# Attention turns the reciprocals of its totals instead of its output and stores x by features

## The chip, the cores and the metric

One core of a Trainium2 chip runs the whole program in one launch. The metric is the device time of that core in microseconds. The engines named below are TensorE (PE in the rows, with PEld for its weight loads), VectorE (DVE), ScalarE (ACT), GpSimd (POOL) and SyncE (SP), which issues most of the DMAs.

## The reference, cut to what matters

Three layers follow one another; each takes the result of the one before.

```python
# attention: q, k, v are (4 batches, 8 heads, 576, 64)
scores = scale * (q @ k.T) + bias            # bias from positions, one map per head
attn = np.exp(scores - scores.max(-1))
attn = attn / (attn.sum(-1) + 1e-09)
out = attn @ v
# dense layer: x is (4*576 = 2304 tokens, 8*64 = 512 features)
x = out.transpose(0, 2, 1, 3).reshape(2304, 512)
h = x @ w_in                                 # 512 -> 2048
x2 = (h - np.tanh(h)) @ w_out                # 2048 -> 512
# experts: each token goes through the one expert of 8 that its gate picks
y = gate * (np.maximum(x2 @ w1[e], 0) @ w2[e])
```

The division by the sum of the exponentials (the *total* of a query and a head) and the layout of x between the first two layers are what this case is about.

## The kernel before

**Attention** works on 16 pairs of heads (g from 0 to 15), and in each on five tiles of queries (t from 0 to 4; four of 128 rows and one of 64), 80 steps in all. In a step TensorE computes the scores of the next tile (`scores`, L412), turns the exponentials of this one (`turn_prob`, L420) and multiplies with v for the pair before (`values`, L427). VectorE adds the bias and finds the maximum of each row (`add_bias`, L644, once for each of the two heads), copies turned exponentials out of PSUM (L713) and splits the next pair's q and k into high and low parts (`low`, L626 and L629). ScalarE takes the exponentials and sums them into `total` (`exponentials`, L563), copies the rest of the turned exponentials (L599, L601) and makes the high parts. There is one PSUM buffer of scores for each head, so `scores` of a tile waits until both `add_bias` of the tile before have read it (`neg_done`, L403 to L405). Each engine carries out its instructions in the order in which they are written.

The output of a pair stands in PSUM with its 128 features on partitions and the 576 queries in columns. VectorE copies it to `o_sb` (`copy_main` at t = 3, L672; `copy_rest` at t = 4, L678). TensorE turns it back tile by tile (`turn_out`, L458), so that queries are on partitions, and VectorE multiplies each turned tile with the reciprocals of the totals while it writes `x_sb` (`scaled`, L664). The reciprocals come from `inverse` (L649 to L654): an addition and a reciprocal on 128 partitions by 10 values (five tiles by two heads), once for each pair, at t = 1 of the pair after it, ahead of `scaled` and of the next `add_bias`. Tile 0 of a pair is turned and scaled at t = 4 of the next pair, and tiles 1 to 4 in steps 0 to 3 of the one after. SyncE stores each pair to `x_dram`, one row for each token (L368, L369).

**The dense layer** takes six chunks of 384 tokens. In each it goes through 16 slots: `up` (L985, 12 matmuls with w_in), an activation shared by ScalarE and VectorE, and `down` (L1042, 9 matmuls with w_out). It needs x with features on partitions, in a high and a low part. So x is loaded by rows (`load_x`, L889), TensorE turns it (`turn_first_x`, L929, for chunk 0 at the end of attention; `turn_x`, L1029, for the others in slots 0, 3 and 6 of the chunk before), and ScalarE and VectorE split it out of PSUM (L934, L939; L1142, L1230). At the change of layers the last pair's `inverse` stands on VectorE ahead of the split of chunk 0, and `first_up` (L989) waits for that split.

**The experts** follow; the change does not touch their arithmetic.

Of the kernel before, what the change touches and what calls it, by code (L numbers as in the profile page):

```python
# [26 lines left out]
P = 128  # L27
# [56 lines left out]
class Dense:  # L84
# [8 lines left out]
    turn_first_x: object  # L93
    split_first_x_high: object
    split_first_x_low: object
# [24 lines left out]
    turned: object  # L120
# [32 lines left out]
def bias_and_attention(nc, stay, mem, w1, b1, w2, dist, psi, rpsi_rows, bias_dram, q, k, v, ident, x_dram):  # L153
# [8 lines left out]

    with ExitStack() as ctx:
# [23 lines left out]
        x_sb = [buf(f"x_sb{i}", [P, QT, 2 * D]) for i in range(2)]  # L187
# [19 lines left out]
        inv = [buf(f"inv{i}", [P, QT, 2]) for i in range(2)]  # L207
# [31 lines left out]
        x4 = x_dram[0:TOK, :].rearrange("(b s) (c e) -> b c s e", b=NB, e=2 * D)  # L239
# [47 lines left out]
        def over(engine):  # L287

            engine.wait_ge(x_done, QT * PAIRS_A)
            for i in range(2):  # L290
                engine.wait_ge(x_out[i], 32 * PAIRS_A // 2)
# [10 lines left out]
        def sync(sp, dense):  # L302
# [45 lines left out]
            for g in range(PAIRS_A + 1):  # L348
# [11 lines left out]
                if g == LASTP:  # L360
                    sp.wait_ge(x_out[LAST_OF_FIRST % 2], 32 * (LAST_OF_FIRST // 2 + 1))
                    dense.load_x(sp, 0)
                    dense.load_second_weights(sp)
                if real(g - 2):
                    p = g - 2
                    sp.wait_ge(x_done, QT * (p + 1))
                    dst = x4[p % NB, p // NB]
                    sp.dma_start(dst[0:MAIN, :].rearrange("(t p) d -> p t d", p=P), x_sb[p % 2][:, 0:QT - 1, :]).then_inc(x_out[p % 2], 16)  # L368
                    sp.dma_start(dst[MAIN:S, :], x_sb[p % 2][0:LAST, QT - 1, :]).then_inc(x_out[p % 2], 16)  # L369
# [4 lines left out]
            sp.wait_ge(x_out[(LAST_OF_FIRST + 1) % 2], 32 * ((LAST_OF_FIRST + 1) // 2 + 1))  # L374
# [3 lines left out]
            dst = x4[p % NB, p // NB]  # L378
            sp.dma_start(dst[0:MAIN, :].rearrange("(t p) d -> p t d", p=P), x_sb[p % 2][:, 0:QT - 1, :]).then_inc(x_out[p % 2], 16)
            sp.dma_start(dst[MAIN:S, :], x_sb[p % 2][0:LAST, QT - 1, :]).then_inc(x_out[p % 2], 16)  # L380
            for i in range(2):
                sp.wait_ge(x_out[i], 32 * PAIRS_A // 2)

        def tensor(pe, dense):
# [94 lines left out]
            for g, t in STEPS:  # L479
# [22 lines left out]
                if turn_of(g, t):  # L502
                    turn_out(*turn_of(g, t), misc, TURN_AT)
# [5 lines left out]
            dense.turn_first_x(pe)  # L509
            misc_free(PAIRS_A, 0)  # L510
            for tile in range(1, QT - 1):
                turn_out(LASTP - 1, tile, misc, tile * P)
            pe.wait_ge(pta_read, QT * PAIRS_A)
            turn_out(LASTP - 1, QT - 1, pt_a, 0)
# [5 lines left out]
            for tile in range(QT - 1):  # L520
                turn_out(LASTP, tile, misc, tile * P)
            turn_out(LASTP, QT - 1, pt_a, 0)

        def scalar(act, dense):
# [83 lines left out]
            for j in range(CH):  # L608
                dense.split_first_x_high(act, j)
            dense.split_second_high(act)  # L610

        def vector(dve, dense):
# [36 lines left out]
            def inverse(p):  # L649
# [4 lines left out]
                nc.vector.reciprocal(inv[p % 2][:, :, :], guarded[:, :, :]).then_inc(norm_step, 1)  # L654

            def scaled(p, tile, tiles, bank, at):
                m = rows(tile)
                if tile <= 1 and p >= 2:
                    dve.wait_ge(x_out[p % 2], 32 * (p // 2))
                dve.wait_ge(norm_step, 2 * p + 2)  # L660
                dve.wait_ge(turn_done, QT * p + tile + tiles)
                by = inv[p % 2][0:m, tile:tile + tiles, :]
                by = bass.AP(by.tensor, by.offset, [by.ap[0], [2, tiles], [1, 2], [0, D]])
                nc.vector.tensor_tensor(x_sb[p % 2][0:m, tile:tile + tiles, :].rearrange("p t (c d) -> p t c d", c=2),  # L664
                                        bank[0:m, at:at + tiles * P].rearrange("p (t c d) -> p t c d", c=2, d=D),
                                        by, ALU.mult).then_inc(x_done, tiles)

            def copy_main(p):
                if p:
                    dve.wait_ge(turn_done, QT * p - 1)  # L670
# [3 lines left out]
            def copy_rest(p, bank, at):  # L674
                if p:
                    dve.wait_ge(turn_done, QT * p)
# [55 lines left out]
            for j in range(CH):  # L732
                dense.split_first_x_low(dve, j)
# [13 lines left out]
CH = 3  # L747
# [25 lines left out]
def dense_and_routing(nc, stay, mem, attention, ctl, first_ctl, slot_i, rows_sb, w_in, w_out, w_gate, before, token_ids, down_order, upto,  # L773
# [4 lines left out]
    with ExitStack() as ctx:  # L778
# [50 lines left out]
        first_turn = [h.rearrange("p (k t) -> p k t", t=P) for h in halves[0:CH]]  # L829
# [7 lines left out]
        x_in = [sem(f"x_in{j}") for j in range(CH)]  # L837
        turned, xt_high, xt_ready = sem("turned"), sem("xt_high"), sem("xt_ready")
# [48 lines left out]
        x_tiles = x_dram[0:TOK, :].rearrange("(c t p) n -> c p t n", p=P, t=CH)  # L887
# [27 lines left out]
        def load_second_x(sp):  # L915
            sp.wait_ge(turned, CH)
# [8 lines left out]
        def turn_first_x(pe):  # L925
            for j in range(CH):
                pe.wait_ge(x_in[j], 16)
                for k in range(KT):
                    last = nc.tensor.transpose(first_turn[j][:, k, :], x_nat[:, j, k * P:(k + 1) * P], id_sb[:, :])  # L929
                last.then_inc(turned, 1)  # L930

        def split_first_x_high(act, j):
            act.wait_ge(turned, j + 1)
            nc.scalar.activation(xt_hi[0][:, :, j * P:(j + 1) * P], first_turn[j][:, :, :], ACT.Copy).then_inc(xt_high, 1)  # L934

        def split_first_x_low(dve, j):
            dve.wait_ge(xt_high, j + 1)
            cols = slice(j * P, (j + 1) * P)
            nc.vector.tensor_tensor(xt_lo[0][:, :, cols], first_turn[j][:, :, :], xt_hi[0][:, :, cols].bitcast(F32),  # L939
# [53 lines left out]
        def sync(sp, experts):  # L993
# [11 lines left out]
            for c in range(CHUNKS):  # L1005
                if c + 2 < CHUNKS:
                    sp.wait_ge(turned, CH * (c + 2))
# [12 lines left out]
        def tensor(pe, experts):  # L1020
            def turn_x(c, j):
                n = c * CH + j
                pe.wait_ge(x_in[j], 16 * (c + 1))
                if n:
                    pe.wait_ge(xt_ready, n)
                if j == 0 and c >= 3:
                    pe.wait_ge(x2_copied, CH * (c - 2))
                for k in range(KT):
                    last = nc.tensor.transpose(turn[:, k, :], x_nat[:, j, k * P:(k + 1) * P], id_sb[:, :])  # L1029
                last.then_inc(turned, 1)  # L1030

# [40 lines left out]
            for m in range(SLOTS):  # L1072
# [5 lines left out]
                j = x_prep(m)  # L1078
                if j is not None:
                    if m == 0:  # L1080
                        attention.turned(pe)
                    turn_x(m // FT + 1, j)
                j = x2_turn(m)
                if j is not None:
                    if j == 0:
                        if m // FT < LATE:
                            pe.wait_ge(xt_ready, CH * (m // FT + 2))
# [51 lines left out]
        def scalar(act, experts):  # L1139
            def split_x(c, j):  # L1140
                act.wait_ge(turned, c * CH + j + 1)
                nc.scalar.activation(xt_hi[c % 2][:, :, j * P:(j + 1) * P], turn[:, :, :], ACT.Copy).then_inc(xt_high, 1)  # L1142

# [877 lines left out]
```

## Time and profile before

| | us |
|---|---|
| median of three runs | 1080.85 |
| lowest and highest | 1079.69, 1084.35 |
| the profiled execution | 1080.45 |
| its span in the trace | 1078.7 |
| TensorE busy | 1037.8 (96%) |
| VectorE busy | 680.2 (63%) |
| ScalarE busy | 626.1 (58%) |

The setup of the bias takes the first 62 us or so, attention goes up to about 356, the dense layer up to about 795 (the first expert's work begins in its last slots), and the experts take the rest. Times in a timeline are microseconds from the start of the span. A value in square brackets behind a row is the time that the engine sat idle before it, and what ended that.

### The profile page before, as it was taken

The page shows a single profiled execution, that of the slowest core. Times are in us where ns is not written, and L with a number is a line of the kernel's source. Part 1 is how long each engine was busy: PE and PEld are TensorE (multiplying, and loading weights), DVE is VectorE, ACT ScalarE, POOL GpSimd, SP SyncE. Part 2 cuts the span into 40 slices and gives each one's busy share as a digit, 9 for nine tenths or more (in the row PEclk, how much of TensorE's full clock was granted, in tenths as well). Part 3 has the DMA queues.
Part 4 walks back from the last instruction along what each step waited for, and adds up shares of the span by engine and source line. Part 5 has one row for each costly group of instructions (what it writes and reads, how often), then busy time and mean ns, then how long its engine had stood idle before and what let it go on. Part 6 is the DMA issues. An engine that isn't in the chain of part 4 may idle for free. (4 is left out here: it accounts for less than half of the span.)

```text
span 1078.7 us, 19176 instructions
## 1 busy us (share of the span) xinstructions
PE 1037.8 (96%) x6642; PEld 819.0 (76%) x6642; DVE 680.2 (63%) x1544; ACT 626.1 (58%) x1331; POOL 91.2 (8%) x134
## 2 busy tenths in 40 slices
PE   5879999999999999999999999999999999999995
PEld 2246666666665899999999999999987888888884
DVE  7967777777787796656657657668753452631410
ACT  6977777777787676655556556556631442622321
POOL 0000000000000000000100100001021331331311
PEclk9999999999999999999999999999989999999998
DMA  6772252431503430000000100201115351531110
GB/s 215 263 243 57 56 177 68 165 84 51 167 24 103 166 108 30 1 30 30 31 1 30 31 1 30 79 30 47 48 40 191 127 200 39 198 110 40 36 47 25
DMA packets 69043, 92.14 MB, mean 85 GB/s; under 512 B 25035, under 2 KB 36683, under 8 KB 68939
## 3 DMA queue, kind: packets, MB, share of 16 engines
q1 hardware_dynamic: 63706, 79.32, 22.5%
q0 software_dynamic: 4192, 11.07, 3.1%
q8 instruction: 51, 0.84, 0.3%
q10 hardware_dynamic: 1056, 0.61, 0.2%
q14 instruction: 38, 0.30, 0.1%
HBM read 66.19 MB, written 25.73 MB: 85 GB/s over the span
## 5 line engine op out<-in xcount | busy, mean ns | idle before, releaser
L985 PE MATMUL score<-dl_xt,dl_weights 128*128 128x384 f32 x1152 | 220.6, 339 | 0.0
L985 PEld LDWEIGHTS score<-dl_xt,dl_weights 128*128 128x128 f32 x1152 | 201.9, 188 | 5.0
L563 ACT ACTIVATE at_prob<-at_neg,at_negmax 128x576 f32<-128x576 f32 (+1 forms) x160 | 123.8, 774 | 52.7 <-DVE at_negmax L644 43.6
L1149 ACT ACTIVATE dl_val<-score 128x384 f32<-128x384 f32 x96 | 47.1, 491 | 145.6 <-PE score L985 144.9
L1239 DVE SCALAR_TENSOR_TENSOR dl_sq<-dl_sq,dl_val 128x384 f32<-128x384 f32 x96 | 53.5, 557 | 111.6 <-ACT dl_sq L1151 111.5
L644 DVE CUSTOM_DVE_ANT_0 at_neg<-score,at_bias 128x576 f32<-128x576 f32 (+1 forms) x160 | 113.9, 748 | 5.6 <-PE score L412 5.3
L1764 PE MATMUL o_acc<-dl_weights,ex_ht_hi 128*128 128x512 f32 (+1 forms) x336 | 108.9, 405 | 1.9 <-DVE ex_ht_lo L1855 1.9
L1733 PE MATMUL score<-dl_weights,ex_xt_hi 128*128 128x512 f32 x336 | 107.3, 401 | 1.4 <-DVE ex_xt_lo L1855 1.4
L427 PE MATMUL o_acc<-at_prob_t,at_v_nat 128*64 128x512 f32 (+1 forms) x320 | 85.7, 616 | 1.2 <-DVE at_o_sb L672 1.2
L1448 POOL DMA_INDIRECT slot_dram<-slot_rows,slot_i x18 | 18.1, 1006 | 750.4 <-DVE slot_i L1320 746.0
L420 PEld LDWEIGHTS pt_b<-id_sb,at_prob 128*128 128x128 f32 (+1 forms) x320 | 32.4, 141 | 63.2 <-ACT at_prob L563 47.8
L1764 PEld LDWEIGHTS o_acc<-dl_weights,ex_ht_hi 128*128 128x128 f32 x336 | 62.5, 191 | 16.0 <-issue 2.1
L1733 PEld LDWEIGHTS score<-dl_weights,ex_xt_hi 128*128 128x128 f32 x336 | 62.7, 192 | 14.0 <-DVE ex_xt_lo L1855 1.8
L1855 DVE TENSOR_TENSOR ex_ht_lo<-pt_b,ex_ht_hi 128x512 fp32r<-128x512 f32 x21 | 14.5, 691 | 89.8 <-ACT ex_ht_hi L1804 89.8
L1816 ACT ACTIVATE ex_y_sb<-o_acc,dl_tile_rows 128x512 f32<-128x512 f32 x21 | 14.4, 688 | 97.1 <-PE o_acc L1764 97.1
L1764 PE MATMUL o_acc<-dl_weights,ex_ht_lo 128*128 128x512 f32 (+1 forms) x168 | 66.8, 398 | 0.0
L1733 PE MATMUL score<-dl_weights,ex_xt_lo 128*128 128x512 f32 x168 | 66.4, 395 | 0.0
L412 PE MATMUL score<-at_k_hi,at_q_hi 64*128 64x288 f32 x320 | 58.6, 342 | 4.8 <-DVE at_negmax L644 3.2
L1042 PE MATMUL o_acc<-dl_weights,dl_g_hi 128*128 128x512 f32 x192 | 60.3, 395 | 2.5 <-DVE dl_g_lo L1230 2.5
L1151 ACT ACTIVATE dl_sq<-dl_val,minus_b 128x384 f32<-128x384 f32 x96 | 59.3, 618 | 3.1
L1042 PE MATMUL score<-dl_weights,dl_g_hi 128*128 128x512 f32 x192 | 59.8, 392 | 0.0
L1250 DVE COPY_PREDICATED dl_sq<-dl_over,dl_big 128x384 f32<-128x384 uint32 x96 | 57.7, 601 | 3.3
(214 smaller groups left out, 2123.5 us busy)
## 6 DMA issues: line engine op xcount, KB each, us to landing
dl_raw<-in_moe_w SPq DMA_DIRECT2D x12, 1024.0 KB, 7.0
ex_raw_b<-in_moe_w SPq DMA_DIRECT2D x8, 1024.0 KB, 6.3
at_bias<-bias_dram SPq DMA_DIRECT2D x3, 2304.0 KB, 10.1
bias_dram<-at_prob SPq DMA_DIRECT2D x20, 288.0 KB, 2.1
at_k_all<-in_k SPq DMA_DIRECT2D x16, 288.0 KB, 3.5
at_q_all<-in_q SPq DMA_DIRECT2D x16, 288.0 KB, 4.3
at_v_nat<-in_v SPq DMA_DIRECT2D x16, 288.0 KB, 3.1
bias_dram<-at_rows_sb SPq DMA_DIRECT2D x16, 288.0 KB, 3.7
```

What stands on the lines that cost most here:

```text
L412: last = nc.tensor.matmul(score[c][:, half, 0:HALF], a[g % 2][part, cols], b[g % 2][part, keys], start=i == 0, stop=i == 2)
L427: last = nc.tensor.matmul(o[c * D:(c + 1) * D, at:at + queries.stop - queries.start], v_nat[g % NV][keys, j, :], prob_t[g % 2][keys, j, qu ...
L563: nc.scalar.activation(prob[n % 2][0:m, c, :], neg[c][n % 2][0:m, :], ACT.Exp, bias=negmax[c][n % 2][0:m, 0:1], scale=-1.0, accum_out=tota ...
L644: nc.vector.tensor_tensor_reduce(out=neg[c][n % 2][0:m, :].rearrange("p (a c) -> p a c", a=2), in0=score[c][0:m, :, 0:HALF], in1=bias[hp % ...
L985: last = nc.tensor.matmul(h_ps[m % NHB][:, 0:CN], w[f // KT][:, k, fc], x[c % 2][:, k, :], start=k == 0 and n == 0, stop=k == KT - 1 and n ...
L1042: last = nc.tensor.matmul(x2_ps[j][:, :], g[m % 2][:, tok], w[f // KT][:, f % KT, :], start=f == 0 and n == 0, stop=f == FT - 1 and n == 2)
L1149: nc.scalar.activation(val[m % 2][:, :], h, ACT.Square).then_inc(act_step, 1)
L1151: nc.scalar.activation(sq[m % 2][:, :], val[m % 2][:, :], ACT.Square, bias=minus_b[:, 0:1], scale=SQ_A).then_inc(sq_done, 1)
L1239: nc.vector.scalar_tensor_tensor(out=sq[m % 2][:, :], in0=sq[m % 2][:, :], scalar=SQ_C, in1=val[m % 2][:, :], op0=ALU.add, op1=ALU.mult).t ...
L1250: nc.vector.copy_predicated(s[:, :], over[m % 2][:, :].bitcast(mybir.dt.uint32), big[m % 2][:, :]).then_inc(dve_step, 1)
L1733: last = nc.tensor.matmul(h_ps[half][:, :], x[:, k, :], w1_of(r, half, w)[:, k, :], start=k == 0 and n == 0, stop=k == KT - 1 and n == 2)
L1764: last = nc.tensor.matmul(y_ps[:, :], x[:, half * KT + k, :], w2_of(half, w, k), start=half == 0 and k == 0 and n == 0, stop=half == 1 and ...
```

## The change

Nothing is turned back any more. `inverse` now reads each of the 10 reciprocals' inputs 64 times and writes them out wide, one for each feature: 128 partitions by 640 values. TensorE turns a tile of those (`turn_inverse`, in the place of `turn_out`), which gives the reciprocals with features on partitions, and `scaled` multiplies `o_sb` with them. `x_sb` and `x_dram` are laid out by features, so a pair is stored with one DMA in rows of 576 values, and a chunk of x is loaded with one DMA already the way the dense layer wants it. `turn_first_x` and `turn_x` are gone, and the splits read the loaded tile in SBUF.

```diff
-        x4 = x_dram[0:TOK, :].rearrange("(b s) (c e) -> b c s e", b=NB, e=2 * D)
+        x4 = x_dram.rearrange("(c e) (b s) -> b c e s", b=NB, e=2 * D)
...
-        inv = [buf(f"inv{i}", [P, QT, 2]) for i in range(2)]
+        inv = [buf(f"inv{i}", [P, QT, 2 * D]) for i in range(2)]
...
-            def turn_out(p, tile, bank, at):
+            def turn_inverse(p, tile, bank, at):
                 if tile == 0:
-                    pe.wait_ge(o_read, p + 1)
-                if tile == QT - 1:
-                    pe.wait_ge(rem_read, p + 1)
+                    pe.wait_ge(norm_step, 2 * p + 2)
                 m = rows(tile)
-                nc.tensor.transpose(bank[0:m, at:at + P], o_sb[:, tile * P:tile * P + m], id_sb[:, :]).then_inc(turn_done, 1)
+                nc.tensor.transpose(bank[:, at:at + m], inv[p % 2][0:m, tile, :], id_sb[0:m, 0:m]).then_inc(turn_done, 1)
...
                 nc.vector.tensor_scalar_add(guarded[:, :, :], total[p % 2][:, :, :], 1e-9).then_inc(norm_step, 1)
                 dve.wait_ge(norm_step, 2 * p + 1)
-                nc.vector.reciprocal(inv[p % 2][:, :, :], guarded[:, :, :]).then_inc(norm_step, 1)
+                one = guarded[:, :, :]
+                many = bass.AP(one.tensor, one.offset, [one.ap[0], [1, 2 * QT], [0, D]])
+                nc.vector.reciprocal(inv[p % 2][:, :, :].rearrange("p t (c d) -> p (t c) d", d=D), many).then_inc(norm_step, 1)
...
+                nc.vector.tensor_tensor(x_sb[p % 2][:, cols], o_sb[:, cols], bank[:, at:at + m], ALU.mult).then_inc(x_done, tiles)
...
             def copy_main(p):
                 if p:
-                    dve.wait_ge(turn_done, QT * p - 1)
+                    dve.wait_ge(x_done, QT * p - 1)
...
         def load_x(sp, c):
-            for j in range(CH):
-                sp.dma_start(x_nat[:, j, :], x_tiles[c, :, j, :]).then_inc(x_in[j], 16)
+            sp.dma_start(x_t, x_dram[:, c * CN:(c + 1) * CN].rearrange("(k p) t -> p k t", p=P)).then_inc(x_in, 16)
...
-        def turn_first_x(pe):
...
+        def split_x_high(act, c, j):
             cols = slice(j * P, (j + 1) * P)
-            nc.vector.tensor_tensor(xt_lo[0][:, :, cols], first_turn[j][:, :, :], xt_hi[0][:, :, cols].bitcast(F32),
+            act.wait_ge(x_in, 16 * (c + 1))
+            if c >= 2:
+                act.wait_ge(h_done, FT * (c - 1))
+            nc.scalar.activation(xt_hi[c % 2][:, :, cols], x_t[:, :, cols], ACT.Copy).then_inc(xt_high, 1)
...
-            def turn_x(c, j):
...
-                    turn_x(m // FT + 1, j)
```

## Rows read from the trace of the kernel before

**Rows 1.** Page, part 1: busy us, share of the span, instructions
```profile
PE 1037.8 (96%) x6642; PEld 819.0 (76%) x6642; DVE 680.2 (63%) x1544; ACT 626.1 (58%) x1331; POOL 91.2 (8%) x134
```

**Rows 2.** Busy time of five engines by stretch, then granted clock, DMA
```profile
84.00:356.00 272.00, 270.24 (x2301) 170.31 (x2298) 210.28 (x617) 202.32 (x562) 0.00 (x0) 1.00 0.34 101
...
380.00:723.00 343.00, 343.00 (x1830) 312.34 (x1829) 226.47 (x462) 206.95 (x418) 9.08 (x9) 1.00 0.09 29
```

**Rows 3.** Timeline, one step with the inverse: start, duration, instruction
```profile
212.21 0.22 DVE L654 RECIPROCAL at_inv<-at_guarded 128x10 f32<-128x10 f32 x1
...
212.34 0.27 DVE L664 TENSOR_TENSOR at_x_sb<-misc,at_inv 128x128 f32<-128x128 f32 x1
...
213.86 0.27 PE L420 MATMUL misc<-id_sb,at_prob 128*128 128x128 f32 x1
213.88 0.08 DVE L644 DVE_READ_ACCUMULATOR2_ANT at_negmax<- 128x1 f32 x1
...
214.07 0.22 PEld L412 LDWEIGHTS score<-at_k_hi,at_q_hi 64*128 64x128 f32 x2 [0.18 <-issue]
```

**Rows 4.** Timeline, the step before it, without an inverse
```profile
210.23 0.08 DVE L644 DVE_READ_ACCUMULATOR2_ANT at_negmax<- 128x1 f32 x1
...
210.67 0.19 PEld L412 LDWEIGHTS score<-at_k_hi,at_q_hi 64*128 64x128 f32 x2 [0.17 <-issue]
```

**Rows 5.** Groups by line and shape, VectorE: count, busy us, mean ns
```profile
L713 DVE COPY at_prob_t<-pt_a 128x512 f32<-128x512 f32 x64 | 43.8, 685 | 0.0
...
L713 DVE COPY at_prob_t<-pt_a 128x256 f32<-128x256 f32 x16 | 6.6, 412 | 0.0
...
L654 DVE RECIPROCAL at_inv<-at_guarded 128x10 f32<-128x10 f32 x16 | 3.5, 217 | 0.5
...
L1306 DVE RECIPROCAL slot_rows<-dl_guarded 128x3 f32<-128x3 f32 x6 | 1.1, 177 | 0.2
...
L1305 DVE TENSOR_SCALAR dl_guarded<-dl_total 128x3 f32<-128x3 f32 x6 | 1.0, 169 | 0.2
```

**Rows 6.** Timeline of TensorE, dense layer: three down steps begin
```profile
450.65 0.63 PE L1042 MATMUL o_acc<-dl_weights,dl_g_hi 128*128 128x512 f32 x2
...
454.84 0.63 PE L1042 MATMUL o_acc<-dl_weights,dl_g_hi 128*128 128x512 f32 x2
...
459.47 0.63 PE L1042 MATMUL o_acc<-dl_weights,dl_g_hi 128*128 128x512 f32 x2
```

**Rows 7.** Groups by line and shape: the turns of x
```profile
L1029 PE MATMUL misc<-id_sb,dl_x_nat 128*128 128x128 f32 x60 | 9.0, 272 | 0.0
```

**Rows 8.** Timeline, the end of attention
```profile
344.44 1.53 PE L929 MATMUL score<-id_sb,dl_x_nat 128*128 128x128 f32 x12
...
345.01 0.21 DVE L678 COPY at_o_sb<-misc 128x64 f32<-128x64 f32 x1
...
347.29 0.22 DVE L654 RECIPROCAL at_inv<-at_guarded 128x10 f32<-128x10 f32 x1
347.43 1.83 DVE L939 TENSOR_TENSOR dl_xt<-score,dl_xt 128x512 fp32r<-128x512 f32 x3
...
350.94 4.43 PE L985 MATMUL score<-dl_xt,dl_weights 128*128 128x384 f32 x24
```

**Rows 9.** Timeline of TensorE near the end, behind an idle stretch
```profile
1061.35 0.73 PE L1764 MATMUL o_acc<-dl_weights,ex_ht_hi 128*128 x2 [1.91 <-DVE ex_ht_lo L1855]
...
1063.08 1.05 PE L1764 MATMUL o_acc<-dl_weights,ex_ht_hi 128*128 x2
```

**Rows 10.** Stretches, columns as in rows 2: two behind idle TensorE
```profile
1060.00:1070.00 10.00, 7.42 (x24) 5.61 (x24) 1.10 (x2) 0.95 (x2) 1.32 (x3) 0.83 0.08 29
...
360.00:362.00 2.00, 1.50 (x7) 1.29 (x8) 1.93 (x5) 1.56 (x5) 0.00 (x0) 1.00 0.30 46
```

**Rows 11.** Timeline, TensorE behind the other idle stretch
```profile
360.50 0.70 PE L1042 MATMUL o_acc<-dl_weights,dl_g_hi 128*128 128x512 f32 x2 [2.47 <-DVE dl_g_lo L1230]
```

**Rows 12.** DMA issues by tile: count, KB each, us to landing
```profile
dl_x_nat<-x_dram SPq DMA_DIRECT2D x18, 256.0 KB, 3.1
```

More of the change, by code:

```diff
@@ L119 @@
     x2_copied: object
-    turned: object
+    xt_ready: object
     scattered: object
@@ L186, in bias_and_attention @@
         bias.append(buf("bias1", [P, QT, 2, S]))
-        x_sb = [buf(f"x_sb{i}", [P, QT, 2 * D]) for i in range(2)]
+        x_sb = [buf(f"x_sb{i}", [P, QT * 2 * D])[:, 0:S] for i in range(2)]
         o_sb = buf("o_sb", [P, S])
@@ L508, in tensor @@
                 pe.wait_ge(neg_done[c], QT * PAIRS_A)
-            dense.turn_first_x(pe)
             misc_free(PAIRS_A, 0)
             for tile in range(1, QT - 1):
-                turn_out(LASTP - 1, tile, misc, tile * P)
+                turn_inverse(LASTP - 1, tile, misc, tile * P)
             pe.wait_ge(pta_read, QT * PAIRS_A)
-            turn_out(LASTP - 1, QT - 1, pt_a, 0)
+            turn_inverse(LASTP - 1, QT - 1, pt_a, 0)
             for slot in range(1, MID + 1):
@@ L520, in tensor @@
             for tile in range(QT - 1):
-                turn_out(LASTP, tile, misc, tile * P)
-            turn_out(LASTP, QT - 1, pt_a, 0)
+                turn_inverse(LASTP, tile, misc, tile * P)
+            turn_inverse(LASTP, QT - 1, pt_a, 0)
         def scalar(act, dense):
@@ L836, in dense_and_routing @@
         slots_cleared = sem("slots_cleared")
-        x_in = [sem(f"x_in{j}") for j in range(CH)]
-        turned, xt_high, xt_ready = sem("turned"), sem("xt_high"), sem("xt_ready")
+        x_in, xt_high, xt_ready = sem("x_in"), sem("xt_high"), sem("xt_ready")
         const_set, ones_set = sem("const_set"), sem("ones_set")
@@ L915, in load_second_x @@
         def load_second_x(sp):
-            sp.wait_ge(turned, CH)
+            sp.wait_ge(xt_ready, CH)
             load_x(sp, 1)
@@ L1020, in tensor @@
         def tensor(pe, experts):
-            def turn_x(c, j):
[L1022 to L1030, printed above, removed]
             def down(m):
@@ L1077, in tensor @@
                 down(m)
[L1078 to L1081, printed above, removed]
-                    turn_x(m // FT + 1, j)
                 j = x2_turn(m)
                 if j is not None:
+                    if m // FT == 1 and j == 0:
+                        attention.turned(pe)
                     if j == 0:
-                        if m // FT < LATE:
-                            pe.wait_ge(xt_ready, CH * (m // FT + 2))
                         pe.wait_ge(x2_read[0], m // FT)
@@ L1647, in first_gather @@
             pool.wait_ge(dense.scattered, 16 * CH * FULL_CHUNKS)
-            pool.wait_ge(dense.turned, NTT)
+            pool.wait_ge(dense.xt_ready, NTT)
             nc.gpsimd.dma_start(early_slots, slot_dram.rearrange("(p n) c -> p n c", p=P)).then_inc(early_slots_in, 16)
```

81 lines of the change are left out of this document (30 added, 51 removed).

## The prediction, made before the changed kernel was run

> **What bounds the kernel now.** I read the page's busy times first: TensorE is busy for 96% of the span, no other engine for two thirds of it [rows 1]. Then the stretches: from 84 to 356 us (attention) TensorE works 270.2 of 272 us, from 380 to 723 us (dense layer) all of the time [rows 2]. So a microsecond taken from TensorE in either stretch is a microsecond of the span, and so is each one in which it has to wait. Then the timeline of one attention step with the inverse, to see how much room VectorE has before TensorE waits. TensorE's last turn of the step starts at 213.86 us, VectorE's second maximum is ready at 213.96 (213.88 + 0.08), and TensorE goes on with the next scores at 214.07 [rows 3]. These scores wait for that maximum, since a head's scores have one buffer. In the step before, the maximum is ready at 210.31 and the scores start at 210.67, a margin of 0.36 us [rows 4]; where the inverse stands the margin is 0.11 us at most. The bracket "issue" of 0.17 and 0.18 us is the same in both, so TensorE does not lose time there yet, but next to nothing is left.
>
> **What the change takes away.** (a) Sixty turns of x in the dense layer, fifteen groups of four [rows 7]. From one down to the next is 4.19 us without such a group (450.65 to 454.84) and 4.63 us with one (454.84 to 459.47) [rows 6]: 0.44 us each, 15 x 0.44 = 6.6 us. TensorE has no idle time in that stretch [rows 2], so all of it counts. (b) The twelve turns of chunk 0, 344.44 to 345.97 us by the rows. They hide another wait: the turns behind them write the bank that VectorE empties until 345.22 (345.01 + 0.21) [rows 8]. The last of the twelve starts at about 345.7 (the group's end less some 0.27 us for one turn), and the others follow it, so about 0.4 us is won, counted under the tail. (c) Two stores and three loads become one each. No compute instruction waits for them now; the loads land in 3.1 us [rows 12] and are issued some nine slots of over 4 us before their use, so I count nothing. For chunk 1 SyncE now waits for the split of chunk 0 instead of its turn; the split of chunk 1 comes over ten us later. Without that cover a late load would cost a few us, once.
>
> **What stays as it was.** TensorE still does five turns for each pair, now of the reciprocals; the last has 64 columns in place of 128, too little to count. `scaled` is still one multiplication over a tile, 0.27 us [rows 3], with one operand in PSUM and one in SBUF. The waits change places but not their weight: `turn_inverse` waits for the inverse of three steps before, and the copies to `o_sb` for products that stand ahead of them on the same engine. The splits are as large as before. I take all this at nothing.
>
> **What it adds: the wide reciprocal.** It goes from 10 to 640 values a partition, 16 times. No row shows a long one, so I bound it. An ordinary copy grows by (685 - 412) / 256 = 1.07 ns a value [rows 5]; at that rate the wide one takes 0.16 + 640 x 0.00107 = 0.84 us. But the two reciprocals of the trace are 217 ns for 10 values and 177 ns for 3, that is 40 / 7 = 5.7 ns a value over a start of 160 ns, while an ordinary operation on 3 values takes 169 [rows 5]. A reciprocal is slow by the value, not by the instruction. That gives 0.16 + 640 x 0.0057 = 3.8 us; with a nanosecond of error in each mean the slope is 5.4 to 6.0 and the result 3.6 to 4.0 us. I take 3.8, as these are rows of the same operation, and keep 0.84 as the lower end. That the input is read with a stride of zero should not matter.
>
> The Trainium skill ("VectorE: DVE Perf Modes", section "First, the fixed hardware budget") says that a reciprocal is an iterative division with a repeat count of 8. If each value took eight passes, the price would be above mine; that is a rival below.
>
> **Where it stands.** In VectorE's order the reciprocal is ahead of `scaled` and of both `add_bias` of the next tile. Behind these wait ScalarE's exponentials (with its copies of turned exponentials queued behind them) and TensorE's next scores; behind the scores everything else of TensorE. The present reciprocal takes 0.22 us, so the delay grows by 3.8 - 0.22 = 3.59 us, less a margin of 0 to 0.11 us [rows 3], say 0.05: 3.54 us of stall. VectorE alone has room (210 of 272 us busy, 60 us more make 270 [rows 2]), but TensorE cannot make good what it lost, being busy in all other steps. Fifteen inverses stand inside attention: 15 x 3.54 = 53.1 us.
>
> **The tail.** The sixteenth stands ahead of the split of chunk 0, for which `first_up` waits. Now it starts at 347.29, the three low parts start at 347.43 and take 1.83 us, and the up starts at 350.94, not held by them [rows 8]. After, with 0.4 us won by (b), the reciprocal starts at 346.9 and ends at 350.7, the split ends at 352.55, the up starts at about 352.65: 1.7 us later.
>
> **The clock.** A stall may also slow TensorE down. Near the end it sits idle for 1.91 us up to 1061.35 [rows 9]; soon after, two matmuls take 1.05 us and the granted clock over ten us is 0.83 [rows 10]. As the two levels are full (2.4 GHz) and half (1.2 GHz), that is 10 x 0.17 = 1.7 us of full-speed work lost. After 2.47 us idle up to 360.50 [rows 11] the clock stayed at 1.00 [rows 10]. So a gap can cost 0 or 1.7 us. The new gaps are longer than both; I take 1.7 for each of fifteen, 25.5 us, and keep 0.
>
> The Trainium skill ("TensorE: Matmul & The Clock Gate", Part 1) says the same in general, that the low clock is the default and activity lifts it; by the 2.47 us gap alone the sum would lack those 25.5 us.
>
> **The sum.** The profiled execution took 1080.45 us, 0.4 below the median of the runs, so no correction. 1080.45 + 53.1 + 25.5 + 1.7 - 6.6 = 1154.2 us.
>
> **The rivals.**
> 1. Stalls, but the clock stays up. For it: the 2.47 us gap. Against: the longer gaps. 1154.2 - 25.5 = 1128.7 us. With a slope of 5.4 ns, 15 x 0.2 = 3 us less, and with a clock that falls in some of the gaps only, anything up to 1154.
> 2. The reciprocal runs at eight passes of 1.07 ns, 8.6 ns a value: 0.16 + 5.5 = 5.6 us, 1.8 us more in each of sixteen places, 29 us: 1183 us. Against it: between 3 and 10 values the duration would have grown by 60 ns, and it grew by 40 [rows 5]. The page on VectorE named above is its ground.
> 3. The cheap reciprocal, and faster. If the wide one takes 0.84 us, a stall is 0.84 - 0.22 = 0.62 us less the margin; with the 0.11 us of the row, 15 x 0.51 = 7.7 against 6.6 + 0.4 won: 1081 us, no change. If VectorE's margin is in truth the 0.36 us of the other steps or more, since it could start its part earlier, the loss is under 15 x 0.26 = 3.9 and the time 1077; at a margin of 0.62 us it is 1073. The point from which it decides is 7.0 / 15 = 0.47 us of delay per inverse: under that the change gains. Against it stand the 5.7 ns a value, and a margin of a third of a microsecond would not rescue a 3.8 us reciprocal.
> 4. The stores and loads of x matter, by lying across rows of x_dram. A chunk that comes late would show as TensorE waiting in the dense layer. Some us at most, in either direction; it moves no case.
>
> **How the numbers follow.** My forecast 0.56, stalls without the clock's fall (or with few) 0.25, eight passes 0.07, cheap with no change 0.08, cheap and faster 0.04. The likeliest gives 1154. The range takes in the first two cases with the bounds of the reciprocal (3.6 us: 1128.7 - 3 = 1125.7, and some stalls may overlap TensorE's own issue gaps, so 1122; 4.0 us and a late start of the clock's rise: 1154 + 3 + 10 = 1167): 1122 to 1168. Left out are the cheap cases and the eight passes, 0.19. A measurement of this kernel can tell 0.5% (5.4 us) from no change: faster 0.04, same 0.07, slower 0.89.
>
> **What would show it.** The row of the reciprocal with 128x640: 3.8 us says the step is right, 0.8 says rival 3, 5.6 rival 2. TensorE's idle time before the scores (L412 before) put down to VectorE's maximum, fifteen times some 3.5 us; the granted clock of the attention stretch, about 0.92 if it falls each time, 1.00 if not. In the dense layer, downs 4.19 us apart throughout, and the layer 6 to 7 us shorter. The first up some 1.7 us later against its attention step. My prediction fails if the 5.7 ns do not hold beyond ten values: everything large hangs on a slope from two short instructions.

## The result, and the profile of the changed kernel

The changed kernel took 1174.7 us (median of three; 1171.99 to 1176.49) against 1081.7 us for the kernel before on the same chip (median of four; 1079.69 to 1084.35): a ratio of 1.0855, 95% interval 1.0815 to 1.0896. (A fourth execution of the changed kernel, disturbed throughout, took 1711.62 us and is left out; with it the median is 1175.6.) The kernel is slower, as forecast, but by more: the forecast was 1154 us, and its range ended at 1168. The profiled execution took 1176.49 us, 96.0 more than that of before, and 22.3 more than the sum of the prediction, which was made against the profiled time.

Busy times of the page of the changed kernel, columns as in [rows 1]:

```profile
PE 1078.1 (92%) x6570; PEld 835.0 (71%) x6570; DVE 743.1 (63%) x1544; ACT 627.4 (53%) x1331; POOL 91.4 (8%) x134
```

TensorE has fewer instructions than before and is busy for longer. That alone says that many of its matmuls ran slowly. Next the groups of the page (line, engine, operation; count, busy us, mean ns; idle time before), and who held TensorE from 84 to 460 us (us in total, times, longest):

```profile
L650 DVE RECIPROCAL at_inv<-at_guarded 128x640 f32<-128x640 f32 x16 | 66.5, 4153 | 0.5
```

```profile
PE misc L453 <- DVE at_x_sb L661: 37.3, 14, 2.7
PE score L408 <- DVE at_negmax L638: 14.1, 15, 3.9
PE score L972 <- DVE dl_xt L926: 2.2, 1, 2.2
PE o_acc L1018 <- DVE dl_g_lo L1197: 2.2, 1, 2.2
```

The wide reciprocal takes 4.15 us. TensorE now waits in two places of each pair, and the larger one isn't ahead of the scores: it is the turn of an inverse into `misc`. The timeline of one pair shows why (start, duration, instruction; in square brackets the idle time before it):

```profile
256.31 4.15 DVE L650 RECIPROCAL at_inv<-at_guarded 128x640 f32<-128x640 f32 x1
...
257.37 0.66 PE L416 MATMUL pt_b<-id_sb,at_prob 128*128 128x128 f32 x4
260.38 0.23 DVE L661 TENSOR_TENSOR at_x_sb<-at_o_sb,misc 128x128 f32<-128x128 f32 x1
260.53 0.74 DVE L638 CUSTOM_DVE_ANT_0 at_neg<-score,at_bias 128x576 f32<-128x576 f32 x1
...
260.76 0.45 PE L453 MATMUL misc<-id_sb,at_inv 128*128 128x128 f32 x1 [2.74 <-DVE at_x_sb L661]
...
261.32 0.78 ACT L557 ACTIVATE at_prob<-at_neg,at_negmax 128x576 f32<-128x576 f32 x1 [4.83 <-DVE at_negmax L638]
...
262.11 0.61 PE L408 MATMUL score<-at_k_hi,at_q_hi 64*128 64x288 f32 x2 [0.69 <-DVE at_negmax L638]
```

`scaled` (L661) reads the turned inverses out of `misc` and stands in VectorE's queue behind the reciprocal. TensorE may not write the next turn into `misc` until it is through, and so waits 2.74 us there; then 0.69 us more for the maximum, which is the wait that the prediction named. ScalarE is idle for 4.83 us in the same queue's shadow.

What the stall does to the clock stands in the stretches (columns as in [rows 2], the granted clock third from the end), first over all of attention, then microsecond by microsecond behind the same stall:

```profile
84.00:440.00 356.00, 303.38 (x2222) 182.59 (x2222) 263.27 (x607) 199.24 (x556) 0.00 (x0) 0.86 0.23 71
...
258.00:260.00 2.00, 0.02 (x1) 0.00 (x0) 2.00 (x1) 0.00 (x0) 0.00 (x0) 1.00 0.91 278
260.00:261.00 1.00, 0.24 (x2) 0.27 (x2) 1.00 (x3) 0.00 (x0) 0.00 (x0) 0.74 0.26 78
261.00:262.00 1.00, 0.42 (x2) 0.01 (x1) 1.00 (x5) 0.68 (x2) 0.00 (x0) 0.50 0.03 14
262.00:263.00 1.00, 0.89 (x8) 0.93 (x10) 0.56 (x1) 1.00 (x6) 0.00 (x0) 0.50 0.00 0
...
266.00:267.00 1.00, 1.00 (x5) 0.21 (x2) 0.09 (x2) 0.00 (x0) 0.00 (x0) 0.50 0.00 0
267.00:268.00 1.00, 1.00 (x6) 0.71 (x5) 0.67 (x1) 0.29 (x1) 0.00 (x0) 0.85 0.00 0
268.00:270.00 2.00, 2.00 (x21) 1.36 (x20) 1.19 (x5) 1.53 (x5) 0.00 (x0) 1.00 0.00 0
```

TensorE has been idle since about 258.0. At about 260.5 the clock falls to half (2.4 to 1.2 GHz) and stays there till about 267.3 (the microsecond from 267 to 268 shows 0.85), for all of the work done in between. From one wide reciprocal to the next are 23.90 us in the middle of attention (232.41, 256.31, 280.21), where before there were 17.51.

Where the 96 us lie, by the starts of the same instructions in both traces (us from the start of the span):

| start of | before | after | added in this part |
|---|---|---|---|
| first inverse's reciprocal | 90.0 | 89.8 | -0.2 |
| sixteenth | 347.3 | 440.7 | +93.7 |
| first up of the dense layer | 350.9 | 446.8 | +2.4 |
| experts' first turn of rows | 786.6 | 879.1 | -3.4 |
| experts' last turn of rows | 1052.7 | 1144.9 | -0.3 |
| end of the span | 1078.7 | 1174.8 | +3.9 |

The dense layer won only 3.4 us of the 6.6. Its slots did become shorter: without turns, downs start 4.19 us apart all through (below, TensorE's timeline). But at its start the clock falls twice, and each fall costs 0.17 x 10 = 1.7 us. The first is around the first up, behind 2.2 us of waiting for the split that the tail's reciprocal delays (L972 in the list above); the second is behind 2.2 us of waiting for the activation (L1018):

```profile
543.31 0.63 PE L1018 MATMUL o_acc<-dl_weights,dl_g_hi 128*128 128x512 f32 x2
...
547.50 0.63 PE L1018 MATMUL o_acc<-dl_weights,dl_g_hi 128*128 128x512 f32 x2
...
551.69 0.63 PE L1018 MATMUL o_acc<-dl_weights,dl_g_hi 128*128 128x512 f32 x2
```

```profile
446.00:456.00 10.00, 8.90 (x41) 8.34 (x41) 6.08 (x11) 3.10 (x6) 0.00 (x0) 0.83 0.35 111
456.00:466.00 10.00, 8.11 (x32) 6.98 (x33) 9.08 (x15) 8.22 (x15) 0.00 (x0) 0.83 0.46 129
466.00:476.00 10.00, 10.00 (x53) 9.21 (x52) 8.45 (x14) 7.42 (x13) 0.00 (x0) 1.00 0.38 110
```

Before, there was no wait at the first up, and one of 2.47 us for the activation left the clock at 1.00 [rows 8, 10, 11]. At the end, the gap ahead of the last downs has grown from 1.91 us [rows 9] to 5.09, and nothing that the trace shows ends it:

```profile
1156.77 1.21 PE L1726 MATMUL o_acc<-dl_weights,ex_ht_hi 128*128 x2 [5.09 <-issue]
```

### The profile page after: what moved, and what is told of

Same layout as the page of the kernel before. It is cut to its first block and busy times, and to the rows that moved or that the text cites. A ratio compares the mean times of both kernels' runs of the same rounds, so it can differ in the third digit from the quotient of the medians.

```text
span 1174.8 us, 19011 instructions
## 1 busy us (share of the span) xinstructions
PE 1078.1 (92%) x6570; PEld 835.0 (71%) x6570; DVE 743.1 (63%) x1544; ACT 627.4 (53%) x1331; POOL 91.4 (8%) x134
## 5 line engine op out<-in xcount | busy, mean ns | idle before, releaser
L972 PE MATMUL score<-dl_xt,dl_weights 128*128 128x384 f32 x1152 | 221.3, 340 | 2.2 <-DVE dl_xt L926 2.2
L972 PEld LDWEIGHTS score<-dl_xt,dl_weights 128*128 128x128 f32 x1152 | 204.6, 190 | 8.5 <-issue 2.3
L423 PE MATMUL o_acc<-at_prob_t,at_v_nat 128*64 128x512 f32 (+1 forms) x320 | 99.2, 704 | 0.3 <-issue 0.3
L416 PEld LDWEIGHTS pt_b<-id_sb,at_prob 128*128 128x128 f32 (+1 forms) x320 | 36.2, 153 | 75.1 <-issue 38.0
L408 PE MATMUL score<-at_k_hi,at_q_hi 64*128 64x288 f32 x320 | 63.0, 373 | 18.2 <-DVE at_negmax L638 17.2
L1817 DVE TENSOR_TENSOR ex_ht_lo<-pt_b,ex_ht_hi 128x512 fp32r<-128x512 f32 x21 | 14.5, 691 | 89.8 <-ACT ex_ht_hi L1766 89.8
L650 DVE RECIPROCAL at_inv<-at_guarded 128x640 f32<-128x640 f32 x16 | 66.5, 4153 | 0.5
L593 ACT ACTIVATE at_prob_t<-pt_b 128x512 f32<-128x512 f32 (+1 forms) x80 | 43.8, 547 | 39.8 <-PE pt_b L416 39.5
L1018 PE MATMUL o_acc<-dl_weights,dl_g_hi 128*128 128x512 f32 x192 | 60.5, 395 | 2.2 <-DVE dl_g_lo L1197 2.2
```

Of the source, the lines that this page charges most:

```text
L408: last = nc.tensor.matmul(score[c][:, half, 0:HALF], a[g % 2][part, cols], b[g % 2][part, keys], start=i == 0, stop=i == 2)
L423: last = nc.tensor.matmul(o[c * D:(c + 1) * D, at:at + queries.stop - queries.start], v_nat[g % NV][keys, j, :], prob_t[g % 2][keys, j, qu ...
L650: nc.vector.reciprocal(inv[p % 2][:, :, :].rearrange("p t (c d) -> p (t c) d", d=D), many).then_inc(norm_step, 1)
L972: last = nc.tensor.matmul(h_ps[m % NHB][:, 0:CN], w[f // KT][:, k, fc], x[c % 2][:, k, :], start=k == 0 and n == 0, stop=k == KT - 1 and n ...
L1018: last = nc.tensor.matmul(x2_ps[j][:, :], g[m % 2][:, tok], w[f // KT][:, f % KT, :], start=f == 0 and n == 0, stop=f == FT - 1 and n == 2)
```

## The experiments

All diffs are against the changed kernel, where nothing else is said. Ratios are against the kernel before on the same chip.

**1. The reciprocal narrow again, GpSimd makes it wide.** The theory: all of the loss hangs on the length of one VectorE instruction. The rival: it comes from the new shape of the work (TensorE turning inverses, stores and loads of x).

```diff
-                one = guarded[:, :, :]
-                many = bass.AP(one.tensor, one.offset, [one.ap[0], [1, 2 * QT], [0, D]])
-                nc.vector.reciprocal(inv[p % 2][:, :, :].rearrange("p t (c d) -> p (t c) d", d=D), many).then_inc(norm_step, 1)
...
+                nc.vector.reciprocal(inv_one[p % 2][:, :, :], guarded[:, :, :]).then_inc(norm_step, 1)
...
+        def gpsimd(pool):
+            for p in range(PAIRS_A):
+                pool.wait_ge(norm_step, 2 * p + 2)
...
+                one = inv_one[p % 2][:, :, :]
+                many = bass.AP(one.tensor, one.offset, [one.ap[0], [1, 2 * QT], [0, D]])
+                nc.gpsimd.tensor_copy(inv[p % 2][:, :, :].rearrange("p t (c d) -> p (t c) d", d=D), many).then_inc(widened, 1)
```

> VectorE takes only the 10 reciprocals again (0.22 us) and GpSimd, idle in attention, copies them out 64 times each; all else is as in the changed kernel. Theory (the 4.15 us reciprocal and the clock that falls in its stall are the whole loss): attention comes back to 17.0 us a pair at a clock of 1.00, and what is left is the gain of the dense layer and of the tail, 1080.5 - 6.6 - 0.4 = 1073.4 us. Rival (the turning of x by features, its stores or its loads cost something too): clearly above 1080. Second rival (GpSimd's copy disturbs VectorE): VectorE's means in attention grow.

Measured: 1080.6 us, ratio 0.9989 (0.9978 to 1.0000). Two groups and attention's stretch:

```profile
L653 DVE RECIPROCAL at_inv_one<-at_guarded 128x10 f32<-128x10 f32 x15 | 3.3, 217 | 0.5
...
L745 POOL COPY at_inv<-at_inv_one 128x640 f32<-128x640 f32 x15 | 10.8, 719 | 325.7 <-DVE at_inv_one L653 325.7
...
84.00:340.00 256.00, 255.63 (x2169) 159.55 (x2168) 199.34 (x593) 192.19 (x542) 10.78 (x15) 1.00 0.32 97
```

The whole loss is gone (1174.7 - 1080.6 = 94 us), with every other part of the change in place: the theory holds for the loss. Of the rival 2 us are left (experiment 7). GpSimd's copies take 0.72 us in nobody's way; VectorE's long operations into `at_neg` keep their mean (749 ns before, 751 here). But the run is 7 us above the 1073.4 that I had expected, and what the change should have won isn't there. From reciprocal to reciprocal it takes 17.68 us against 17.51 before (not 17.0, as the expectation has it); the dense layer won 4.9 us rather than 6.6, for the clock fell behind a wait of 2.21 us (0.83 from 360 to 370 us, the same 1.7 us); and the gap at the end was 5.29 us. Experiments 7 and 8 follow these up.

**2. The reciprocal narrow, VectorE makes it wide by a copy.** A middle dose: a delay of under a microsecond on the same engine at the same place.

```diff
-                one = guarded[:, :, :]
...
+                nc.vector.reciprocal(inv_one[:, :, :], guarded[:, :, :]).then_inc(norm_step, 1)
+                dve.wait_ge(norm_step, 3 * p + 2)
+                one = inv_one[:, :, :]
                 many = bass.AP(one.tensor, one.offset, [one.ap[0], [1, 2 * QT], [0, D]])
-                nc.vector.reciprocal(inv[p % 2][:, :, :].rearrange("p t (c d) -> p (t c) d", d=D), many).then_inc(norm_step, 1)
+                nc.vector.tensor_copy(inv[p % 2][:, :, :].rearrange("p t (c d) -> p (t c) d", d=D), many).then_inc(norm_step, 1)
```

> VectorE takes the 10 reciprocals and then copies them out to 640 values, so the wide write stays and the wide division goes. Copy 0.16 + 640 x 0.00107 = 0.84 us, in VectorE's order at the place of the reciprocal. Theory: a stall of about 0.8 us a pair with no fall of the clock, 15 x 0.8 = 12, less 7: about 1085 us. Rival (the margin of VectorE is larger than read, 0.4 us or more): 1079 or less. Rival (writing wide is what costs): near the changed kernel, 1175.

Measured: 1088.2 us, ratio 1.0066 (1.0048 to 1.0084). Its copy's group, and TensorE's wait:

```profile
L653 DVE COPY at_inv<-at_inv_one 128x640 f32<-128x640 f32 x14 | 6.9, 494 | 0.5
...
PE score L409 <- DVE at_negmax L639: 7.3, 14, 0.5
```

The copy costs 0.49 us, and TensorE waits 0.5 us for the maximum, fourteen times; from reciprocal to reciprocal are 18.22 us, 0.54 more than in experiment 1. So all of a delay on VectorE goes through, in line with the small margin of the prediction (0 to 0.11 us). With so short a stall the clock stays at 1.00 in attention, and the waiting is at the scores alone. The copy itself was cheaper than the 0.84 us by the slope of [rows 5].

**3. The wide reciprocal in the kernel before.** The converse of 1: nothing of the change but the long instruction, its result read by nobody. The diff is against the kernel before.

```diff
                 nc.vector.reciprocal(inv[p % 2][:, :, :], guarded[:, :, :]).then_inc(norm_step, 1)
+                one = guarded[:, :, :]
+                many = bass.AP(one.tensor, one.offset, [one.ap[0], [1, 2 * QT], [0, D]])
+                nc.vector.reciprocal(unused[:, :, :].rearrange("p t (c d) -> p (t c) d", d=D), many)
```

> The kernel before, with the wide reciprocal added behind the narrow one; its result is not read. One part of the change alone. Theory (the wide reciprocal and what follows from it are the whole loss of attention): a pair of 23.9 us at a clock of 0.86 as in the changed kernel, and none of the gains: 1176 + 7 = 1183 us, or some us more as the narrow reciprocal stays (15 x 0.2). Rival (the turning of the reciprocals or the copies' new waits take part): clearly less, under 1170.

Measured: 1178.7 us, ratio 1.0913 (1.0894 to 1.0932). TensorE's waits, and the stretch:

```profile
PE misc L459 <- DVE at_x_sb L668: 38.4, 14, 2.9
PE score L413 <- DVE at_negmax L645: 14.3, 15, 4.0
...
84.00:440.00 356.00, 302.80 (x2242) 184.55 (x2240) 266.74 (x626) 200.44 (x556) 0.00 (x0) 0.87 0.24 71
```

The same two waits and the same clock as after the change. The instruction alone is enough for the loss.

**4. TensorE's stall filled, one step too early.** To part the stall from the clock: 24 more turns into `pt_b` (of the same values, so the output stays), in the step whose VectorE work holds the reciprocal. If the clock stays up, its price is seen by itself.

```diff
-                for j in range(MID + 1, KTP):
-                    last = turn_prob(pt_b, (j - MID - 1) * P, n, j)
+                for again in range(7 if t == 1 and g >= 2 else 1):
+                    for j in range(MID + 1, KTP):
+                        last = turn_prob(pt_b, (j - MID - 1) * P, n, j)
```

> The changed kernel, but in each step with the wide reciprocal TensorE repeats its four turns into pt_b seven times (24 more turns, about 2.7 us) before it signals them, in the time in which it would stand idle; VectorE's work is unchanged. Theory (each idle stretch costs a second time through the clock, some 3.1 us): granted clock of attention 1.00, a pair 20.8 us instead of 23.9, 1176 - 46 = 1130 us. Rival (the pair is as long as VectorE's chain makes it, the clock costs nothing of its own): no change, 1172 to 1180.

Measured: 1202.9 us, ratio 1.1124 (1.1099 to 1.1149). A miss. TensorE's waits in it, from 84 to 440 us:

```profile
PE misc L453 <- DVE at_x_sb L662: 35.6, 13, 2.7
PE score L408 <- DVE at_negmax L639: 15.3, 14, 3.9
```

The stall is where it was and as long. VectorE's step t = 1 runs beside TensorE's next one, so the turns came ahead of the stall: they made each pair some 2.5 us longer (24 turns of 0.11 us are 2.6) and filled nothing. The run says nothing on the clock's price, but shows in which step the stall lies.

**5. The same turns, one step later.** `t == 2 and g >= 1` in place of `t == 1 and g >= 2`; nothing else.

> The changed kernel with the repeated turns one step later, in step t = 2, where the trace shows TensorE idle for 2.7 us ahead of its turn of the reciprocals and then 0.7 us ahead of the scores; 24 more turns fill the 2.7. VectorE's work is unchanged. Theory (the clock costs about 3 us a pair of its own): clock of attention 1.00, a pair 17.1 + 3.9 = 21.0 us instead of 23.9, 15 pairs: 1176 - 44 = 1132 us, although TensorE does more. Rival (the stall alone sets the pair): 1172 to 1180.

Measured: 1138.7 us, ratio 1.0534 (1.0516 to 1.0552). Attention's stretch, and TensorE's waits there:

```profile
84.00:410.00 326.00, 308.93 (x2616) 203.93 (x2614) 266.04 (x610) 199.29 (x556) 0.00 (x0) 1.00 0.26 80
...
PE score L408 <- DVE at_negmax L639: 13.6, 15, 1.3
PE misc L453 <- DVE at_o_sb L674: 1.0, 1, 1.0
```

Here the reciprocal still takes 4.15 us on the same queue, and TensorE does 24 x 0.11 = 2.6 us more work in a pair. Still the kernel is some 35 us faster than the changed one (ratios 1.0534 and 1.0855). The wait at `misc` for `scaled` has turned into work (the 1.0 us left is another, at the end of attention, which the changed kernel has too), the clock stays at 1.00, and from reciprocal to reciprocal are 21.56 us in place of 23.90. The only thing taken away is TensorE's idle time, and with it the fall of the clock. So of the 93.7 us that attention lost, 316.4 - 257.3 = 59.1 (first to sixteenth reciprocal, here and before) are the reciprocal's delay, and 351.0 - 316.4 = 34.6 are the clock, 2.3 for each of fifteen stalls. I had expected 1132 us, some 7 less, mostly since I took 17.1 us for a pair of before: 17.51 + 3.93 is 21.4, not 21.0, and fifteen pairs make 6 us of it.

**6. The reciprocal in five parts, and in two.** About the same VectorE work, but each stall much shorter, in the hope that the clock stays up; then stalls of a middle length.

```diff
+            def wide_part(p, tile):
...
+                one = guarded[:, tile, :]
+                many = bass.AP(one.tensor, one.offset, [one.ap[0], [1, 2], [0, D]])
+                nc.vector.reciprocal(inv[p % 2][:, tile, :].rearrange("p (c d) -> p c d", d=D), many).then_inc(norm_step, 1)
...
+                if t and real(g - 1):
+                    wide_part(g - 1, t - 1)
+                if t == 0 and real(g - 2):
+                    wide_part(g - 2, QT - 1)
```

> The wide reciprocal in five parts of 128 values, one in each step, ready before they are turned. VectorE's work is the same or 0.6 us a pair more, but no stretch of it is long. Each part 0.16 + 128 x 0.00625 = 0.96 us, less a margin of 0.36 us in most steps: 3.0 to 4.3 us a pair lost, clock 1.00. Theory (stall plus clock): 1080.5 - 6.6 + 15 x 3.0 to 4.3 + 2 = 1121 to 1140 us. Rival (only the sum of VectorE's work counts): as the changed kernel, about 1175. Rival (VectorE's idle 0.77 us a step hides the parts): under 1095.

Measured: 1116.3 us, ratio 1.0329 (1.0303 to 1.0354), a little under the 1121 to 1140 that I had expected. For the two parts, three tiles at t = 1 and two at t = 3 in the same way:

> The wide reciprocal in two parts, three tiles (384 values) at t = 1 and two (256) at t = 3. By 6.25 ns a value the parts take 2.6 and 1.8 us, so TensorE stands idle for about 2.2 and 1.4 us a pair, the same loss in sum as with one (3.6 us against 3.8). Theory (the clock falls when TensorE stands idle for long at a time): if 2.2 us are short enough, clock 1.00 and 1080.5 - 4 + 15 x 3.6 = 1131 us; if they are not, with a loss of 1.7 us each, 1156 us. Rival (the same stall costs the same however it is cut): 1175 us.

Measured: 1137.0 us, ratio 1.0493 (1.0446 to 1.0540), between the 1131 of a clock that stays up and the 1156 of one that falls each time. First the five parts (group, wait of TensorE, stretch), then of the two parts the groups, TensorE's two waits behind the first part in two pairs in a row, and the stretches of three pairs in a row, each from one pair's first reciprocal to the next:

```profile
L653 DVE RECIPROCAL at_inv<-at_guarded 128x128 f32<-128x128 f32 x63 | 59.7, 947 | 0.4
...
PE score L408 <- DVE at_negmax L637: 29.1, 56, 0.8
...
84.00:380.00 296.00, 265.07 (x2211) 164.23 (x2211) 260.03 (x661) 190.65 (x550) 0.00 (x0) 1.00 0.28 85
```

```profile
L653 DVE RECIPROCAL at_inv<-at_guarded 128x384 f32<-128x384 f32 x12 | 30.6, 2553 | 1.2
L653 DVE RECIPROCAL at_inv<-at_guarded 128x256 f32<-128x256 f32 x11 | 19.2, 1746 | 0.0
...
138.28 0.30 PE L452 MATMUL misc<-id_sb,at_inv 128*128 128x128 f32 x1 [1.16 <-issue]
...
139.67 0.44 PE L408 MATMUL score<-at_k_hi,at_q_hi 64*128 64x288 f32 x2 [0.98 <-DVE at_negmax L637]
...
160.41 0.30 PE L452 MATMUL misc<-id_sb,at_inv 128*128 128x128 f32 x1 [1.16 <-issue]
...
161.80 0.40 PE L408 MATMUL score<-at_k_hi,at_q_hi 64*128 64x288 f32 x2 [0.98 <-DVE at_negmax L637]
...
112.10:135.48 23.38, 20.95 (x153) 12.54 (x152) 17.56 (x42) 13.15 (x39) 0.00 (x0) 0.85 0.18 52
135.48:157.61 22.13, 19.67 (x153) 11.98 (x152) 17.56 (x42) 13.05 (x39) 0.00 (x0) 0.92 0.37 125
157.61:178.40 20.79, 18.14 (x153) 11.11 (x152) 17.47 (x43) 12.93 (x39) 0.00 (x0) 1.00 0.36 111
```

In five parts VectorE does slightly more than after the change (5 x 0.95 = 4.7 us a pair in place of 4.15), and still 58 us are back (1174.7 - 1116.3): the stalls are 0.5 us on average (29.1 / 56), each step's own margin is used [rows 4], and the clock doesn't fall in attention. In two parts TensorE waits 1.16 and 0.98 us behind the first part in nearly every pair, and a pair takes 20.8, 22.1 or 23.4 us all the same. The three sorts differ in the clock: 1.00 in the pair of 20.8 us, 0.92 in that of 22.1 and 0.85 in that of 23.4, which are 0, 1.8 and 3.5 us of full-speed work lost. So a fall can be of two sizes, and the larger one makes a pair 2.6 us longer, near the 2.3 us of experiment 5, which is a second measure of the clock's price. The same two waits stood ahead of a fall in one pair and of none in the next, so it isn't the length of the wait alone that decides, and no run shows what does.

**7. The last tile turned whole.** Experiment 1 left 0.17 us a pair (17.68 against 17.51). The suspect: the fifth turn, of 64 rows, which the prediction had counted as free. The diff is against experiment 1; the lower 64 rows that are now turned are read by nobody.

```diff
-                m = rows(tile)
-                nc.tensor.transpose(bank[:, at:at + m], inv[p % 2][0:m, tile, :], id_sb[0:m, 0:m]).then_inc(turn_done, 1)
+                nc.tensor.transpose(bank[:, at:at + P], inv[p % 2][:, tile, :], id_sb[:, :]).then_inc(turn_done, 1)
```

> As the one in which GpSimd widens, but the fifth tile of the reciprocals is turned whole, 128 rows instead of 64 (the lower 64 are reciprocals of ones that nobody reads). Theory (turning 64 rows between turns of 128 costs TensorE 0.13 us each time, 2.1 us in all): attention 2 us shorter, 1078.5 us. Rival (the 2 us of attention came from something else, such as GpSimd beside VectorE): 1080.6 as before.

Measured: 1078.8 us, ratio 0.9977 (0.9966 to 0.9987). The reciprocals are 17.51 us apart again, to the hundredth the figure of before, and from the first to the sixteenth are 257.1 us instead of 259.1. A turn of half the rows cost more than a whole one. In TensorE's timelines the 64-row turn of experiment 1 starts 0.58 us after the four turns before it do and the next instruction 0.21 us after it; with the whole turn these are 0.49 and 0.11. Why isn't shown. Of the dense layer's start this run shows one thing more:

```profile
360.33 1.08 PE L1029 MATMUL o_acc<-dl_weights,dl_g_hi 128*128 128x512 f32 x2 [2.46 <-DVE dl_g_lo L1208]
```

```profile
360.00:364.00 4.00, 3.67 (x9) 2.92 (x10) 3.78 (x8) 3.58 (x7) 0.00 (x0) 0.57 0.28 60
```

The wait is as long as before [rows 11], and here the clock did fall behind it.

**8. Code moved along.** In experiments 1 and 2 and after the change the gap at the end was above 5 us, in experiment 7 it was 4.60, in experiments 4 to 6, whose programs for TensorE are longer, 2.5 or 2.6, all put down to "issue". The suspect is the fetch of instructions, if its timing hangs on where in the program the last downs lie. The edit, against experiment 7, makes TensorE wait ahead of each of the five turns of a pair rather than the first alone; the four more are always met. (No run shows the 1024 bytes that the expectation speaks of.)

```diff
-                if tile == 0:
-                    pe.wait_ge(widened, p + 1)
+                pe.wait_ge(widened, p + 1)
```

> As e6_whole_last_turn, but TensorE waits for GpSimd at each of the 80 turns and not at 16; the waits are met long before, and TensorE's program is longer by 1024 bytes, as that of the five parts was. Theory (the 5.3 us in which TensorE waits for nothing ahead of its last matmuls is the loading of its next instructions and depends on where they lie): that gap goes to about 2.5 us, and the time to 1078.5 - 2.8 = 1075.7 us. Rival (the gap has another cause): it stays at 5.3 us and the time at that of e6_whole_last_turn.

Measured: 1075.5 us, ratio 0.9956 (0.9941 to 0.9971). The last downs of experiment 7, and of this one:

```profile
1059.02 1.22 PE L1737 MATMUL o_acc<-dl_weights,ex_ht_hi 128*128 x2 [4.60 <-issue]
```

```profile
1056.00 0.73 PE L1736 MATMUL o_acc<-dl_weights,ex_ht_hi 128*128 x2 [2.79 <-issue]
```

This version is faster than both kernels, by 0.4% against before. The gap has shrunk by 1.8 us, and the clock, which had fallen in it (1.22 us for the two matmuls), was up (0.73). That waits which are always met, hundreds of microseconds earlier, change the gap speaks for the fetch of code; no view shows the fetch itself, so this cause is supported and not shown.

## Why the prediction was right or wrong

**What bounds the kernel: right.** A delay on VectorE ahead of the scores' maximum reaches the end whole: 0.49 us gave 0.5 us of waiting at each of fourteen places (experiment 2), and the instruction alone made the loss (experiment 3).

**The dense layer's gain: right in its terms, 3.2 us short.** Downs are 4.19 us apart without turns, as worked out. What I took over unasked was the clock of before at the layer's start: behind 2.47 us of waiting for the activation it had stayed up, and it fell behind 2.2 us after the change and in experiment 1, and behind 2.46 in experiment 7. And the stall of the tail, which I had priced at 1.7 us, got no fall of the clock in my sum, though each of the other fifteen did. 2 x 1.7 = 3.4 us went back so.

**The wide reciprocal: a term mis-sized.** 4.15 us for 3.8, above my 4.0. The slope over the long ones is (4153 - 947) / 512 = 6.3 ns a value, where two short ones had given 5.7 (between 3 and 10 values). My bound allowed for rounding of the two means, and not that a straight line through 3 and 10 need not hold to 640. The Trainium skill ("VectorE: DVE Perf Modes", section "First, the fixed hardware budget") gives a repeat count of 8; with the 1.07 ns of copies out of PSUM I had made 8.6 ns of it, rival 2, and the measured 6.3 excludes that. As an estimate by that page's count, eight passes of 0.78 ns would give it; no run here shows the length of a pass. The cheap reciprocal (rival 3) was wrong by 3.3 us an instruction.

**The stall: right in its working, wrong in place.** The delay added is 4.15 - 0.22 = 3.93 us, less a margin near 0.1: 3.8 for each. With the fifth turn's 0.13 that is 59 us for fifteen, as experiment 5 shows (59.1). I had 53.1. I named the scores as the wait and passed over `misc`, four fifths of it (2.74 of 3.43 us), though I had written that `scaled` stood in the same queue. Under "what stays as it was" I let this wait keep its weight. Experiment 4 missed for the same reason: I hadn't drawn which step of TensorE runs beside which of VectorE.

**The clock: the term that failed most.** I took 1.7 us from a fall behind a gap of 1.91 us. The fall in attention lasts about twice as long (24 us at 0.86 are 3.4 us of full-speed work, against 10 x 0.17). It costs 2.3 us net, 34.6 in fifteen places for 25.5; a part of it costs nothing, as the clock is already low in the last of the stall (260.5 to 262.1 us in the timeline, with some 1 us of idle time). The Trainium skill ("TensorE: Matmul & The Clock Gate", Part 1) has the low clock as the default that activity lifts, and the trace agrees: it fell while TensorE stood still and stayed low for some 7 us, most of them full of work. Rival 1, the clock staying up at 1128.7 us, did not come: the clock stayed up only where the gaps were filled, and that kernel takes 1138.7 (experiment 5).

**The fifth turn: a step that failed.** What I had called "too little to count" cost 2.0 us (experiment 7). **The tail: right.** From the sixteenth reciprocal to the first up 2.4 us more, where 0.4 + 1.7 = 2.1 were worked out. The 0.4 us won ahead of it can't be told from the rest. **The transfers: right.** No compute waits for x's loads, rival 4 is empty. **The end: not foreseen.** 3.9 us behind the experts' last turn, of which the gap is 3.2.

Together, against the sum: clock in attention 9.1, reciprocal 15 x 0.3 = 4.5, fifth turn 2.0, dense layer 3.2, end 3.9, tail 0.3: 23.0, with the experts' -0.3 22.7, of 22.3 us. The direction needed none of these. The range failed by the sum of several terms, the clock's first, since I let 3.6 to 4.0 us and one size of the clock's fall stand for what I hadn't seen.

## What to carry to other kernels

Widen a small result by a copy and not by computing it wide: 640 reciprocals on VectorE cost 4.15 us, ten and a copy 0.7, and with the copy on an idle GpSimd a pair took no longer than before (17.51 us, experiment 7). Before putting a long instruction on a queue whose results a busy TensorE awaits, list every buffer that waits behind it, since the first wait may be for a buffer that is to come free and not for a result. Where such a stall can't be avoided, cut it into pieces: in five parts the kernel took 58 us less than in one, though still some 35 more than before.

## What the runs showed of the hardware that I had not expected

- A reciprocal on VectorE over n values a partition took 176 ns (3), 217 (10), 947 (128), 1746 (256), 2553 (384), 4153 (640).
- A gap's length by itself did not decide the clock: 2.47 us left it up before, 2.46 us at the same place did not in experiment 7, nor 2.2 us after; behind the same 1.16 and 0.98 us some pairs of the two-part version lost 3.5 us of full-speed work, some 1.8 and some none. Waits of 0.8 us and less in attention never did it here, and the stalls of 2.74 us at `misc` always.
- Executions of one kernel differ in their clock too: the seventeen of the kernel before that ran beside experiments 1 and 2 reach from 1078.7 us at a mean granted clock of 0.991 to 1084.46 at 0.984. So a single fall of 1.7 us in one trace may be that execution's own.
- A 64-row turn among 128-row ones made a pair 0.17 us longer than a whole one did (17.68 against 17.51).
- A gap near the end, put down to nothing that the trace shows, was 5.1 to 5.4 us in three programs, 4.6 in one and 2.5 to 2.8 in five whose programs for TensorE are longer, and the version with waits added was the fastest of all.
